# A gated scan with two feed-forward layers: block 1 of layer 1 in seven products, and the making of layer 2's output weights moved one phase on

## The chip, the cores and the metric

The kernel runs on one core of one Trainium2 chip. The metric is device microseconds of one execution, median of several runs; lower is better. A kernel has five engines here: TensorE (PE, matmuls), VectorE (DVE), ScalarE (ACT), GpSimd (POOL), and SyncE (SP), which only issues DMAs. Each engine runs its own instruction stream in order, and semaphores tie the streams together.

## The reference

```python
def _attn_ref(x, f_logit, lower_bound):            # x, f_logit: [2, 6080, 256]
    sig = 1.0 / (1.0 + np.exp(-f_logit))
    f = lower_bound + (1.0 - lower_bound) * sig
    i = 1.0 - f
    for t in range(S):
        h = f[:, t] * h + i[:, t] * x[:, t]
        y[:, t] = h
    return y
def _moe_ref(x, w_in, w_out):                      # w_in [256, 2048], w_out [2048, 256]
    h = np.maximum(x @ w_in, 0.0)
    return h * h @ w_out
def _moe2_ref(x, w_in, w_out):
    h = x @ w_in
    g = np.where(h > 0.0, h, np.exp(np.minimum(h, 0.0)) - 1.0)
    return g @ w_out
# reference = _moe2_ref(_moe_ref(_attn_ref(...).reshape(12160, 256)))
```

## The kernel before, in words

**Tiles.** Time is cut into blocks of 512 steps (11 full blocks and a tail of 448), for both batches at once. Block i of layer 1 is `first(i)`, block n of layer 2 `second(n)`. Each is a phase; phases run in the order first(0), first(1), second(0), first(2), second(1) and so on. Their number is `ph.order`: phase zero is first(0), phase one first(1), phase two second(0), phase three first(2). A phase has 8 pairs (`PAIRS`), each of 256 of the 2048 hidden columns; a pair is a step of the phase.

**Precision.** Each fp32 operand is split into a high part (a rounding copy on ACT) and a low part (a subtraction on DVE or POOL). A product of a 128x128 weight tile with 128x512 data is three matmuls (`triple`, L600 to L605).

**Two ways to multiply up.** The first matmul of a layer takes 2x2 tiles of weights to 2x2 tiles of data. A plain phase (`plain()`, before: phases zero and one) does it in 8 triples a step, 24 matmuls. All others use seven products in the manner of Strassen and Winograd: m1 to m7, 21 matmuls (L688 to L731), with four sums of weights (s1 to s4), which are kept in DRAM and loaded for each pair (`load_sums`, `load_s`), and four sums of the data (t1 to t4). The products land in four PSUM banks (`ring`) and are combined: ACT copies m1 (L1096) and m2 (L1104) out, DVE adds m6, m7, m5, m3 and m4 (L1439 to L1464), and POOL adds m1 to m2's copy (c11, L1747). The second matmul of the layer (`down`) has 8 triples, 24 matmuls, for the pair two steps back, into `acc`. In a phase of seven products, PE alternates product and down: m1, down, m2, down, m6, down, m7, down, m5, down, m3, down, m4, down, down.

**After the products.** Of the pair one step back, ACT does the activation of the half n1 (`n1_of`), then of n0 (`relu_of_n0`, `act_of_n0`), then the high parts (`hi_of_n1` L1075, `hi_of_n0` L1085); DVE the low parts (`lo_of`, L1414). In an ACT step the order is: place a, copy of m1, n1_of, place b, relu_of_n0, copy of m2, act_of_n0, hi_of_n1, place c, hi_of_n0, place d. The places take hosted work for other phases: gates, splits of the next inputs, and the preparation of the weights.

**Preparation of the weights**, once, in phases zero and one. For each pair, SP loads the four quarters of w_in, ACT and DVE split them (`quarters_hi` L922, `quarters_lo` L1316), POOL makes four sums (`sums`, L1591 to L1596), ACT takes their high parts (`sums_hi_of`, L929, place b), POOL their low parts (`sums_lo_of`, L1601), and SP stores all to DRAM. Layer 1's run in phase zero, layer 2's in phase one. The output weights are split on ACT (`weights_hi_out`, L941 and L944) and DVE (`weights_lo_out`); layer 1's stay in SBUF, and layer 2's go to DRAM and are loaded for each pair.

**What holds POOL.** Its add of m1 and m2 (c11, L1747) stands behind `pool.wait_ge(lo_n1, cur.g)`: it waits for DVE's low part of n1 of the pair one step back. ACT's relu_of_n0 of the next step waits for c11, and PE's m3 for the copy of m2 (`pe.wait_ge(m2_kept, cur.s + 1)`).

Of the kernel before, what the change touches and what calls it, by code (L numbers as in the profile page):

```python
# [11 lines left out]
P = 128  # L12
# [3 lines left out]
PAIRS = 8  # L16
# [18 lines left out]
def gated_scan_two_ffn(nc, x, f_logit, lower_bound, w_in1, w_out1, w_in2, w_out2, out):  # L35
# [20 lines left out]
    class Phase:  # L56
# [9 lines left out]
        def plain(self):  # L66
            return isinstance(self.order, int) and self.order < 2

    PLAIN = 2 * PAIRS
# [45 lines left out]
    with ExitStack() as ctx:  # L115
# [122 lines left out]
        q_loaded = [sem(f"q_loaded{v}") for v in range(2)]  # L238
# [90 lines left out]
        def wr_count(layer, p):  # L329
            return W_LOADS[1] * (p // 2 + 1) if layer == 1 else W_LOADS[1] * PAIRS // 2 + W_LOADS[2] * (p + 1)  # L330
# [27 lines left out]
        def _(sp):  # L358
# [45 lines left out]
            def load_raw_out(layer, p):  # L404
# [9 lines left out]
                sp.wait_ge(w_lo, PAIRS - 1 if p == 0 else v)  # L414
                sp.dma_start(o, wout2_v[:, 2 * p:2 * p + 2, :]).then_inc(wr_loaded[0], DMA_INC)
# [68 lines left out]


            QUARTER_AT = {1: 1, 4: 2, 5: 3}

            def phase(ph, after):
# [8 lines left out]
                for p in range(PAIRS):  # L497
                    g = ph.base + p
                    nxt = ahead(p + 2)
                    if known(ph.order, 0):  # L500
                        if p == PAIRS - 1:
                            load_q(ahead(p + 1))
                        if p >= 1:
# [10 lines left out]
                            if p + 3 < PAIRS:  # L514
                                load_raw_in(1, p + 3)
                            elif p + 3 < PAIRS + 2:
                                load_raw_in(2, p + 3 - PAIRS)
                        continue
                    if known(ph.order, 1):
                        if p < PAIRS - 1:  # L520
                            load_q(ahead(p + 1))
                        else:
                            load_s(ahead(p + 1))
                            load_sums(ahead(p + 1))
                        if 1 <= p < PAIRS - 1:
# [9 lines left out]
                        if p in QUARTER_AT:  # L535
                            load_f(2, QUARTER_AT[p])
                            load_x(2, QUARTER_AT[p])
                        continue
                    if known(ph.order, 2) and p == 0:
                        load_s(ahead(1))  # L540
                        load_sums(ahead(1))
                    if known(ph.order, 2) and p == 0:
                        keep_sums(2, PAIRS - 1)
# [1262 lines left out]
```

## Time and profile before

| | |
|---|---|
| Median of 3 runs | 1975.05 us (1974.92 to 1975.56) |
| The profiled execution's own time | 1975.2 us |
| Its span, first to last instruction | 1973.4 us |
| PE busy | 1963.1 us (99%), 8734 matmuls |
| DVE, ACT busy | 1574.9 us (80%), 1511.6 us (77%) |
| POOL busy | 608.8 us (31%) |
| PE's granted clock | 0.999 of full speed over the span |
| PE's part in the chain that ended last | 98% |

Busy PE time overlaps (a matmul's 0.39 us reaches into the next), so the pace of PE is read from the starts of its rows. In the rows of the timeline the first number is the start in us from the span's start, the second the time to the end of the row's last instruction. Phase one begins at about 91.5 us, phase two at 178.5, phase three at 260.1 (from the first row of a phase's matmuls and the pace).

### The profile page before, as it was taken

Reading aid. Unit: us, or ns where it says so; the run is one execution under the profiler, and the core shown is the slowest. Engines: PE = TensorE matmul, PEld = TensorE weight load, DVE = VectorE, ACT = ScalarE, POOL = GpSimd, SP = SyncE. Lnnn points to the kernel's source line nnn. Section 1 sums busy time; section 2 is a strip of 40 time slices with the busy share of each in tenths; the row PEclk is TensorE's granted clock in tenths of the full one; section 3 lists DMA queues with packets and bytes.
Section 4 is the critical chain, followed back from the end, with each engine's and each line's share of the span. In section 5 each row is a group of like instructions: output and inputs, shape, how many; then the busy total and the mean of one; then the engine's idle time right before and its main releaser. Section 6 shows DMA issues by size and latency. Waiting matters only on the chain.

```text
span 1973.4 us, 27926 instructions
## 1 busy us (share of the span) xinstructions
PE 1963.1 (99%) x8734; PEld 1636.4 (83%) x8734; DVE 1574.9 (80%) x1775; ACT 1511.6 (77%) x1826; POOL 608.8 (31%) x506
## 2 busy tenths in 40 slices
PE   8999999999999999999999999999999999999998
PEld 6888888888888888888888888888888888888888
DVE  6656888888888888788888888878888877866887
ACT  7888778778777777777777777778777777767766
POOL 3454323323233232332322323223232232322410
PEclk9999999999999999999999999999999999999999
DMA  6668444444444444354444444434444443443453
GB/s 181 198 213 275 147 147 115 148 137 128 136 146 136 128 137 137 114 157 146 125 129 138 133 137 146 139 107 147 143 125 147 141 126 113 142 133 118 140 172 111
DMA packets 229635, 283.09 MB, mean 143 GB/s; under 512 B 153729, under 2 KB 166018, under 8 KB 229506
## 3 DMA queue, kind: packets, MB, share of 16 engines
q1 hardware_dynamic: 226832, 280.49, 46.4%
q10 hardware_dynamic: 2674, 1.25, 0.2%
q8 instruction: 36, 0.59, 0.1%
q14 instruction: 93, 0.76, 0.1%
HBM read 249.30 MB, written 32.37 MB: 143 GB/s over the span
## 4 chain that ended last, share of the span: by engine, by line
PE 98%; ACT 0%; DMA 0%; DVE 0%; POOL 0%; issue 0%; ACTq 0%; DVEq 0%
PE acc L604 52%; PE ring L604 46%; DMA xb<-in_x_dram 0%; PE acc L756 0%; POOL ee L1601 0%; POOL o_sb L1596 0%; DVE wout L1323 0%; DVE y_raw L1496 0%; ACT xb L1017 0%; ACT hid_hi L1075 0%; ACT xb L1012 0%; ACT xa L1017 0%; DVE t_lo L1502 0%; ACT t_hi L1150 0%; DVE y_raw L1488 0%
## 5 line engine op out<-in xcount | busy, mean ns | idle before, releaser
L604 PE MATMUL acc<-hid_hi,wout 128*128 128x512 f32 (+1 forms) x3072 | 1142.4, 387 | 1.2 <-DVE wout L1323 0.7
L604 PE MATMUL ring<-t_hi,s_w 128*128 128x512 f32 (+1 forms) x2720 | 1035.2, 387 | 1.4 <-DVE t_lo L1502 1.4
L604 PEld LDWEIGHTS acc<-hid_hi,wout 128*128 128x128 f32 x3072 | 576.7, 188 | 115.4 <-issue 1.1
L604 PEld LDWEIGHTS ring<-t_hi,s_w 128*128 128x128 f32 x2720 | 510.6, 188 | 103.4 <-DVE t_lo L1502 1.6
L604 PE MATMUL acc<-hid_lo,wout 128*128 128x512 f32 (+1 forms) x1536 | 594.7, 387 | 0.0
L604 PE MATMUL ring<-t_lo,s_w 128*128 128x512 f32 (+1 forms) x1360 | 526.6, 387 | 0.0
L1747 POOL TENSOR_TENSOR xb<-xb,m_sb 128x512 f32<-128x512 f32 (+1 forms) x176 | 225.7, 1282 | 965.1 <-DVE hid_lo L1414 962.8
L1096 ACT ACTIVATE m_sb<-ring 128x512 f32<-128x512 f32 (+1 forms) x176 | 104.4, 593 | 363.6 <-PE ring L604 345.0
L604 PEld LDWEIGHTS acc<-hid_lo,wout 128*128 128x128 f32 x1536 | 288.4, 188 | 56.5
L604 PEld LDWEIGHTS ring<-t_lo,s_w 128*128 128x128 f32 x1360 | 255.3, 188 | 50.4
L1414 DVE TENSOR_TENSOR hid_lo<-xa,hid_hi 128x1024 fp32r<-128x1024 f32 (+1 forms) x191 | 230.7, 1208 | 82.5 <-ACT hid_hi L1075 82.4
L1414 DVE TENSOR_TENSOR hid_lo<-xb,hid_hi 128x1024 fp32r<-128x1024 f32 (+1 forms) x191 | 241.5, 1264 | 30.4 <-ACT hid_hi L1085 30.4
L1085 ACT ACTIVATE hid_hi<-xb 128x1024 fp32r<-128x1024 f32 (+1 forms) x191 | 200.1, 1048 | 37.5 <-DVE xb L1408 37.0
L1456 DVE TENSOR_TENSOR xa<-ring,u_sb 128x1024 f32<-128x1024 f32 (+1 forms) x176 | 211.9, 1204 | 0.0
L1408 DVE SCALAR_TENSOR_TENSOR xa<-ee,xa 128x1024 f32<-128x1024 f32 (+1 forms) x95 | 115.4, 1215 | 104.9 <-ACT ee L1042 104.9
L1075 ACT ACTIVATE hid_hi<-xa 128x1024 fp32r<-128x1024 f32 (+1 forms) x191 | 198.7, 1040 | 0.5
L1439 DVE TENSOR_TENSOR u_sb<-ring,m_sb 128x512 f32<-128x512 f32 (+1 forms) x176 | 118.4, 673 | 44.1 <-PE ring L604 43.1
L1445 DVE TENSOR_TENSOR u_sb<-ring,u_sb 128x512 f32<-128x512 f32 (+1 forms) x176 | 120.6, 685 | 40.6 <-PE ring L604 28.8
L1408 DVE SCALAR_TENSOR_TENSOR xb<-ee,xb 128x1024 f32<-128x1024 f32 (+1 forms) x95 | 114.9, 1209 | 26.4 <-ACT ee L1065 26.4
L1460 DVE TENSOR_TENSOR xa<-ring,xa 128x512 f32<-128x512 f32 (+1 forms) x176 | 120.7, 686 | 18.3
L1464 DVE TENSOR_TENSOR xb<-ring,u_sb 128x512 f32<-128x512 f32 (+1 forms) x176 | 118.0, 670 | 0.0
L1042 ACT ACTIVATE ee<-ee 128x1024 f32<-128x1024 f32 (+1 forms) x95 | 100.2, 1054 | 3.0
(122 smaller groups left out, 1706.5 us busy)
## 6 DMA issues: line engine op xcount, KB each, us to landing
s_w<-s_kept SPq DMA_DIRECT2D x184, 512.0 KB, 3.8
s_w<-s_kept SPq DMA_DIRECT2D x176, 384.0 KB, 4.1
wout<-w_kept SPq DMA_DIRECT2D x96, 512.0 KB, 4.4
out_dram<-o_sb SPq DMA_DIRECT2D x88, 128.0 KB, 3.5
f_raw<-in_f_logit_dram SPq DMA_DIRECT2D x168, 64.0 KB, 3.5
x_raw<-in_x_dram SPq DMA_DIRECT2D x168, 64.0 KB, 2.7
s_kept<-ee SPq DMA_DIRECT2D x16, 512.0 KB, 5.2
s_kept<-s_w SPq DMA_DIRECT2D x8, 512.0 KB, 3.9
```

The source lines that it names most:

```text
L604: mm = nc.tensor.matmul(out_ap, lhs[a], rhs[b], start=start and t == 0, stop=stop and t == 2)
L1075: nc.scalar.activation(hid_hi[:, pr.par(), 0:2, 0:N], xa[:, pr.par(), :, 0:N], ACT.Copy).then_inc(hi_n1, 1)
L1085: nc.scalar.activation(hid_hi[:, pr.par(), 2:4, 0:N], xb[:, pr.par(), :, 0:N], ACT.Copy).then_inc(hi_n0, 1)
L1096: nc.scalar.activation(m1_sb[:, 0:N], bank("m1", cur), ACT.Copy).then_inc(m1_kept, 1)
L1408: nc.vector.scalar_tensor_tensor(out=x2, in0=ee[:, v, :, 0:pr.N], scalar=1.0, in1=x2, op0=ALU.subtract, op1=ALU.max).then_inc(done, 1)
L1414: nc.vector.tensor_tensor(hid_lo[:, pr.par(), k:k + 2, 0:N], x2, hid_hi[:, pr.par(), k:k + 2, 0:N].bitcast(F32), ALU.subtract).then_inc(do ...
L1439: nc.vector.tensor_tensor(u[:, 0], bank("m6", cur), m1_sb[:, 0:N], ALU.add).then_inc(u2_done, 1)
L1445: nc.vector.tensor_tensor(u[:, 1], bank("m7", cur), u[:, 0], ALU.add).then_inc(u3_done, 1)
L1456: nc.vector.tensor_tensor(t, bank("m5", cur).unsqueeze(1).broadcast_to([P, 2, N]), u, ALU.add).then_inc(u4_done, 1)
L1460: nc.vector.tensor_tensor(t[:, 0], bank("m3", cur), t[:, 0], ALU.add).then_inc(c12_done, 1)
L1464: nc.vector.tensor_tensor(x_n0(cur)[:, 1], bank("m4", cur), u[:, 1], ALU.add).then_inc(c21_done, 1)
L1747: nc.gpsimd.tensor_tensor(t, t, m1_sb[:, 0:N], ALU.add).then_inc(c11_done, 1)
```

## The change

- Phase one, first(1), is no longer plain: its up matmuls are seven products with the loaded sums of layer 1. Its data sums t1 to t4 are made in phase zero, on POOL, their high parts there on ACT (5c, 6b, 6c), and their low parts on DVE (`lo_b1` to `lo_tb1`) instead of POOL. Phase zero's second scan of a quarter moves from place c to b.
- Phase one loads sums and quarters (`load_s`, `load_sums`) as other phases do; `load_q` is gone.
- Layer 2's sums stay in phase one, but on POOL they now stand behind c11: in step p, c11, one hosted operation for the next phase, the low parts of sums p, then the sums of pair p + 1. The hosted operations for second(0) move one pair later (`crowded`).
- Layer 2's output weights are split in phase two: ACT at place a, POOL (no longer DVE) ahead of c11, stored by SP. Down matmuls of phase two use them in their place, without a load. Layer 2's quarters take that tile (`wout2`) in phase one.

The pieces below are, in order: which phases are plain and where layer 2's quarters lie; TensorE; SyncE in phase zero; ScalarE; GpSimd.

```diff
         def plain(self):
-            return isinstance(self.order, int) and self.order < 2
+            return isinstance(self.order, int) and self.order < 1
...
         def q2_new(p):
-            t = (t_lo if p % 2 else t_hi)[1]
-            return t[:, 4:6, :].rearrange("p v s -> p (v s)").rearrange("p (x h m) -> p x h m", h=2, m=P)
+            return wout2[:, p % 2].rearrange("p j h d -> p (j h d)").rearrange("p (x h m) -> p x h m", h=2, m=P)
...
             plain_phase(first(0))
-            plain_phase(first(1))
...
+            phase(first(1))
             phase(second(0))
...
-                        if p == PAIRS - 1:
-                            load_q(ahead(p + 1))
...
+                        if p >= PAIRS - 2:
+                            load_s(nxt)
+                            load_sums(nxt)
...
+                    crowded = known(ph.order, 1)
...
                 if known(ph.order, 1):
                     if place == "a":
                         quarters_hi(2, p)
                     if place == "b":
                         sums_hi_of(2, p)
-                    if place == "d" and p < PAIRS - 1:
-                        weights_hi_out(2, p)
+                if known(ph.order, 2) and place == "a" and p >= 1:
+                    weights_hi_out(2, p - 1)
...
                 if ph.plain():
...
+                    sums(1, p)
+                    if p == 6:
+                        sum_t1(first(1))
+                        sum_t3(first(1))
+                        sum_t2(first(1))
+                        sum_t4(first(1))
+                    sums_lo_of(1, p)
+                    if p == PAIRS - 1:
+                        sums(2, 0)
                     return
-                if nxt is not None and 2 <= p < 7:
+                nxt = inputs_of(ph)
+                crowded = known(ph.order, 1)
+                if nxt is not None and 2 <= p < (8 if crowded else 7):
...
+                if known(ph.order, 2) and p >= 1:
+                    weights_lo_out(p - 1)
...
                 pool.wait_ge(lo_n1, cur.g)
...
                 nc.gpsimd.tensor_tensor(t, t, m1_sb[:, 0:N], ALU.add).then_inc(c11_done, 1)
                 if nxt is not None:
-                    if p == 1:
+                    if p == (2 if crowded else 1):
                         lo_b(nxt)
...
+                if crowded:
+
+                    sums_lo_of(2, p)
+                    if p < PAIRS - 1:
+                        sums(2, p + 1)
```

How the streams move. First POOL in phase one, at pair 2 (before; `o_sb` holds the raw quarters and sums, `ee` the stored form, `z_raw` the data of phase two):

```order
L1594 TENSOR_TENSOR o_sb<-o_sb 128x128 [waits sums_done]
L1596 TENSOR_TENSOR o_sb<-o_sb 128x128 [waits sums_done]
L1615 TENSOR_TENSOR t_lo<-z_raw,t_hi 128x512 [waits t_hb]
L1658 TENSOR_TENSOR z_raw<-z_raw 128x512 [waits t_lb]
L1601 TENSOR_TENSOR ee<-o_sb,ee 128x4x128 [waits sums_hi]
L1591 TENSOR_TENSOR o_sb<-o_sb 128x128 [waits r_loaded1]
```

The same place in the changed kernel, from c11 of pair 2 to c11 of pair 3:

```order
L1723 TENSOR_TENSOR xb<-xb,m_sb 128x512 [waits m1_kept,m2_kept,lo_n1,m6_done]
L1608 TENSOR_TENSOR t_lo<-z_raw,t_hi 128x512 [waits t_hb]
L1594 TENSOR_TENSOR ee<-o_sb,ee 128x4x128 [waits sums_hi]
L1584 TENSOR_TENSOR o_sb<-o_sb 128x128 [waits r_loaded1]
L1585 TENSOR_TENSOR o_sb<-o_sb 128x128
L1587 TENSOR_TENSOR o_sb<-o_sb 128x128 [waits sums_done]
L1589 TENSOR_TENSOR o_sb<-o_sb 128x128 [waits sums_done]
L1642 TENSOR_TENSOR z_raw<-z_raw 128x512 [waits t_lb,m6_done]
L1723 TENSOR_TENSOR xb<-xb,m_sb 128x512 [waits m2_kept,m1_kept,lo_n1]
```

The sums of a pair (L1584 to L1589) now come after the c11 of the pair before, with its wait on lo_n1, one hosted operation and the low parts.

ACT in phase one, at pair 3, before:

```order
L922 ACTIVATE t_lo1<-o_sb 128x3x128 [waits s2_stored1,r_loaded1]
L1012 ACTIVATE xa<-ring 128x1024 [waits lo_n1,up_n1]
L1017 ACTIVATE xa<-xa 128x1024 [waits relu_n1]
L1075 ACTIVATE hid_hi<-xa 128x1024 [waits down_n1,acted_n1]
L929 ACTIVATE ee<-o_sb 128x4x128 [waits sums_stored1,sums_done]
L1012 ACTIVATE xb<-ring 128x1024 [waits lo_n0,up_n0]
```

and in the changed kernel:

```order
L896 ACTIVATE wout2<-o_sb 128x3x128 [waits s2_stored1,r_loaded1]
L1074 ACTIVATE m1_sb<-ring 128x512 [waits c11_done,u2_done,m1_done]
L1008 ACTIVATE xa<-xa 128x1024 [waits c12_done,u4_done]
L1010 ACTIVATE xa<-xa 128x1024 [waits relu_n1]
L903 ACTIVATE ee<-o_sb 128x4x128 [waits sums_stored1,sums_done]
L1029 ACTIVATE xb<-xb 128x1024 [waits c21_done,c11_done]
L1082 ACTIVATE xb<-ring 128x512 [waits lo_n0,m2_done]
```

The copy of the sums (L903, waits for sums_done from POOL) stands ahead of the copy of m2 (L1082), for which PE's m3 waits.

## Rows read from the trace of the kernel before

**Rows 1.** Waits of PE, whole span (waited for: us in total, times, longest).

```profile
PE ring L604 <- DVE t_lo L1502: 1.4, 1, 1.4
...
PE acc L604 <- DVE hid_lo L1414: 0.5, 1, 0.5
```

**Rows 2.** Busy time by window (stretch, its length, each engine): phases one, three.

```profile
91.50:178.50 87.00, 87.00 (x385) 72.05 (x384) 50.77 (x56) 71.75 (x95) 53.71 (x52) 1.00 0.73 239
...
260.10:341.70 81.60, 81.60 (x361) 67.57 (x361) 68.07 (x79) 65.02 (x80) 24.42 (x19) 1.00 0.45 129
```

**Rows 3.** PE timeline, phase three: m1 and m3 of a step, the next m1.

```profile
280.56 0.39 PE L604 MATMUL ring<-t_hi,s_w 128*128 128x512 f32 x1
...
287.36 0.39 PE L604 MATMUL ring<-t_hi,s_w 128*128 128x512 f32 x1
...
290.76 0.39 PE L604 MATMUL ring<-t_hi,s_w 128*128 128x512 f32 x1
```

**Rows 4.** Timeline of ACT in phase three, two steps.

```profile
285.88 0.57 ACT L1104 ACTIVATE xb<-ring 128x512 f32<-128x512 f32 x1
...
287.30 1.04 ACT L1075 ACTIVATE hid_hi<-xa 128x1024 fp32r<-128x1024 f32 x1
...
305.33 1.04 ACT L1051 ACTIVATE xb<-xb 128x1024 f32<-128x1024 f32 x1
306.28 0.58 ACT L1104 ACTIVATE xb<-ring 128x512 f32<-128x512 f32 x1
```

**Rows 5.** Timeline of DVE in phase three.

```profile
288.38 1.22 DVE L1414 TENSOR_TENSOR hid_lo<-xa,hid_hi 128x1024 fp32r<-128x1024 f32 x1 [1.57 <-ACT hid_hi L1075]
...
294.41 1.83 DVE L1291 TENSOR_TENSOR_SCAN y_raw<-gate,carry,x_t 128x256 f32<-128x256 f32 x1
```

**Rows 6.** Timeline of POOL in phase three.

```profile
289.68 1.30 POOL L1747 TENSOR_TENSOR xb<-xb,m_sb 128x512 f32<-128x512 f32 x1 [4.18 <-DVE hid_lo L1414]
290.93 1.30 POOL L1629 TENSOR_TENSOR t_lo<-z_raw,t_hi 128x512 fp32r<-128x512 f32 x1
294.40 1.30 POOL L1629 TENSOR_TENSOR t_lo<-z_raw,t_hi 128x512 fp32r<-128x512 f32 x1 [2.17 <-PE ring L604]
```

**Rows 7.** Timeline of POOL in phases zero and one: low parts and sums.

```profile
61.82 1.29 POOL L1601 TENSOR_TENSOR ee<-o_sb,ee 128x512 fp32r<-128x512 f32 x1 [7.41 <-ACT ee L929]
...
64.83 0.46 POOL L1596 TENSOR_TENSOR o_sb<-o_sb 128x128 f32<-128x128 f32 x1
...
140.97 2.26 POOL L1601 TENSOR_TENSOR ee<-o_sb,ee 128x512 fp32r<-128x512 f32 x1
...
145.25 0.80 POOL L1596 TENSOR_TENSOR o_sb<-o_sb 128x128 f32<-128x128 f32 x1
...
158.09 1.81 POOL L1601 TENSOR_TENSOR ee<-o_sb,ee 128x512 fp32r<-128x512 f32 x1 [0.66 <-ACT ee L929]
...
161.24 1.44 POOL L1596 TENSOR_TENSOR o_sb<-o_sb 128x128 f32<-128x128 f32 x1
```

**Rows 8.** Timeline of DVE in phase one.

```profile
161.14 1.23 DVE L1414 TENSOR_TENSOR hid_lo<-xb,hid_hi 128x1024 fp32r<-128x1024 f32 x1 [2.39 <-ACT hid_hi L1085]
...
165.73 0.54 DVE L1316 TENSOR_TENSOR t_hi<-o_sb,t_hi 128x384 fp32r<-128x384 f32 x1
...
174.38 0.74 DVE L1291 TENSOR_TENSOR_SCAN y_raw<-gate,carry,x_t 128x256 f32<-128x256 f32 x1
```

**Rows 9.** Timeline of ACT, pair 0 of phase one: copy of sums, then relu.

```profile
102.99 0.61 ACT L929 ACTIVATE ee<-o_sb 128x512 fp32r<-128x512 f32 x1
103.51 1.01 ACT L1012 ACTIVATE xb<-ring 128x1024 f32<-128x1024 f32 x1
```

**Rows 10.** Timeline of ACT where phase one ends and two begins.

```profile
181.81 1.06 ACT L1085 ACTIVATE hid_hi<-xb 128x1024 fp32r<-128x1024 f32 x1
182.77 0.58 ACT L1096 ACTIVATE m_sb<-ring 128x512 f32<-128x512 f32 x1
```

**Rows 11.** Timeline of POOL in phase two, a c11 with its idle time.

```profile
217.67 1.30 POOL L1747 TENSOR_TENSOR xb<-xb,m_sb 128x512 f32<-128x512 f32 x1 [2.30 <-DVE hid_lo L1414]
```

More of the change, by code:

```diff
@@ L460, in load_s @@
                 v = pr.par()
-                if known(pr.phase.order, 2):
-                    sp.wait_ge(s2_stored[v], DMA_INC * (pr.p // 2 + 1))
+                if isinstance(pr.phase.order, int) and pr.phase.order < 3:
+                    sp.wait_ge((s1_stored if pr.layer == 1 else s2_stored)[v], DMA_INC * (pr.p // 2 + 1))
                 if isinstance(pr.s, int) and pr.s < 2:
@@ L534, in phase @@
                             keep_sums(2, p - 1)
[L535 to L543, printed above, removed]
+                    if known(ph.order, 2):
+                        if 1 <= p < PAIRS - 1:
+                            load_raw_out(2, p + 1)
+                        if p == 0:
+                            keep_sums(2, PAIRS - 1)
+                        else:
+                            keep_w2(p - 1)
+                    if known(ph.order, 3) and p == 0:
+                        keep_w2(PAIRS - 1)
+                        for v in range(2):
+                            sp.wait_ge(w2_stored[v], DMA_INC * PAIRS // 2)
                     if ph.layer == 1 and not known(ph.i, TAIL):
@@ L842, in set_free @@
             def set_free(ph):
-                if isinstance(ph.order, int) and ph.order < 4:
-                    act.wait_ge(up_n0, ph.base - PAIRS)
-                else:
+                if known(ph.order, 2):
+                    act.wait_ge(up_n0, PLAIN)
+                elif not known(ph.order, 1):
                     act.wait_ge(m4_done, ph.base - PAIRS - PLAIN)
@@ L854, in raw_of @@
                 return z_raw if ph.layer == 2 else y_raw
-            def split_plain_b(ph):
-                raw_ready(ph, False)
-                nc.scalar.activation(t_hi[ph.order % 2][:, 0:4:3, :], raw_of(ph)[:, 0], ACT.Copy).then_inc(t_hb, 1)
             def split_b(ph):
@@ L972, in hosted @@
                 if nxt is not None:
-                    late = ph.plain() or (ph.layer == 2 and known(ph.i, TAIL - 1))
+                    crowded = known(ph.order, 1)
+                    late = crowded or (ph.layer == 2 and known(ph.i, TAIL - 1))
                     if at == ((2, "c") if late else (1, "b")):
@@ L989, in hosted @@
                         tanh(ph.i + 1, 2)
-                    if at == (7, "d") and not ph.plain():
+                    if at == (7, "d"):
                         tanh(ph.i + 1, 3)
-                if known(ph.order, 2):
-                    if at == (0, "c"):
-                        tanh(2, 3)
-                    if at == (0, "d"):
-                        weights_hi_out(2, PAIRS - 1)
                 if known(ph.order, 1):
```

249 lines of the change are left out of this document (108 added, 141 removed).

## The prediction

> **What bounds the kernel now.** I read the waits of PE first, then the busy time by window, then the timelines of single steps. PE waits for others six times in the whole span, all in the first 28 us: the longest is 1.4 us, the shortest shown 0.5 [rows 1]. From there to the end PE is never late: in both windows it is busy for the full stretch, 87.00 of 87.00 and 81.60 of 81.60 us [rows 2]. So every matmul taken away counts, and so does every wait that appears. A step of seven products is 45 matmuls and takes 290.76 - 280.56 = 10.20 us, 0.2267 us a matmul [rows 3]. PE's granted clock is 1.00 in both windows [rows 2], the 2.4 GHz level.
>
> **The gain.** Phase one goes from 48 to 45 matmuls in each of 8 steps: 24 x 0.2267 = **5.4 us less** on PE, and 4390 matmuls stand in the written stream (loop body once) where 4414 did. This counts in full only if the others keep a step of 10.20 us in phase one. Nothing else on PE changes.
>
> **Who has to keep up, and how late they may be.** PE issues m3 287.36 - 280.56 = 6.80 us into a step [rows 3], and m3 waits for ACT's copy of m2. That copy starts at 285.88, 5.32 us in, and takes 0.57 [rows 4], so it may start at 6.23 and has 0.9 us to spare. What matters in phase one is thus the return time R, from the start of one copy of m2 to the next. If R is over 10.20, PE waits the difference at each m3.
>
> **R in the changed phase one.** POOL's sums of pair p + 1 now come after c11 of pair p, and ACT takes them ahead of the copy of m2. So a loop closes through three engines. Its terms:
> - From the copy of m2 to c11. ACT goes on to the high part of n1 (287.30), DVE makes the low part (288.38, 1.22 us), and c11, which waits for it, starts at 289.68 [rows 4 to 6]: 289.68 - 285.88 = 3.80.
> - c11 itself: 290.93 - 289.68 = 1.25 to the next start [rows 6].
> - One hosted operation for phase two, in five of the seven turns (pairs 2 to 6): 1.27, near the 1.30 of rows 6.
> - Low parts of sums p and sums p + 1, five instructions. Three instances: 61.82 to 65.29 = 3.47; 158.09 to 162.68 = 4.59; 140.97 to 146.05 = 5.08 [rows 7].
> - ACT's copy of the sums to its next instruction 0.52 [rows 9], 0.08 for the semaphores, relu_of_n0 to the copy of m2 306.28 - 305.33 = 0.95 [rows 4].
>
> Which of the three instances holds is decided by what DVE does at that time. In rows 5 and 6 a scan and a POOL low part start together at 294.4: POOL's takes its usual 1.30, the scan 1.83 where one takes 0.74 alone [rows 8]. In the instance of 4.59, the last sum takes 1.44 where one takes 0.46 in the first instance, exactly beside DVE's low part at 161.14 [rows 7, 8]. So the two exclude each other, whole instructions at a time. In the changed loop DVE makes the low part of n0 right in this window (1.23), and in pairs 2, 4 and 6 the scans (0.74 each) fall in it too; the quarters (0.54) come near its end [rows 8]. I take 4.6 for pairs 3 and 5, the instance with such overlap, and 4.6 + 0.7 = 5.3 for 2, 4 and 6, near the worst instance. The Trainium skill (SBUF — State Buffer, Who interferes with whom) has a rule for this: a DVE instruction with two SBUF inputs and a GpSimd instruction that reads SBUF exclude each other, and whoever starts first holds the port. By that rule the sum is the one taken here; if they only shared a bandwidth, or not at all, it would be the first rival's below. The trace agrees with the rule at 294.4.
>
> R = 3.80 + 1.25 + 1.27 + 4.6 + 0.08 + 0.52 + 0.95 = 12.5 us for pairs 3 and 5, and 13.2 for 2, 4 and 6. Five turns: 2 x 12.5 + 3 x 13.2 = 64.6 us, where PE's five steps need 51.0. **Excess 13.6 us.**
>
> **Slack before it starts.** Pairs 0 to 2 have no hosted operation behind c11 ahead of them. The copy of m2 in pair 2 starts at 5.32 less the one hosted copy in that step (0.95) plus the copy of the sums 0.52, plus 0.7 because ACT's second copy of `acc` must wait for the end of PE's step 1 and the quarters' copy follows: about 5.6, slack 6.23 - 5.6 = 0.6 us. **Less 0.6.**
>
> **Start of phase one.** Where phase one ends today, ACT's copy of m1 comes 0.96 after hi_of_n0 starts, at 182.77 [rows 10], and ends at 183.35; PE wants it for m5 at 178.5 + 24 x 0.2267 = 183.9. In the changed kernel, two copies stand between them at the start of phase one, some 0.5 + 0.4. That makes it 0.4 late. **Plus 0.4.**
>
> **Edits at nothing.** The work for t1 to t4 in phase zero: POOL had 7.41 us idle ahead of its row at 61.82 [rows 7], and the four sums (4 x 1.3) take the place of three low parts of about the same time; ACT gets two copies of 0.95 and gives one back, over a phase with plain matmuls to wait for. If that cover is gone, the first m5 and m6 of phase one are late. Weights in phase two: ACT's two copies fall where it waits for the next m1. POOL's two subtractions of 256 elements, between 0.45 and 1.30 each by size [rows 6, 7], about 1.5 in all, have 2.30 us idle ahead of c11 [rows 11]. Bounds are 0 and 0.4 a step (both delayed by a DVE instruction of 1.2), and a late c11 has room: it ends at 290.98, 0.2 into the next step, and ACT's relu_of_n0 wants it at 285.88 - 0.95, 4.4 into one [rows 3, 4, 6]. So 0. SP: eight `load_q` go, eight loads each of sums and quarters come; they land in about 4 us and are asked for a step ahead. SP's wait on w_lo stands ahead of the next loads in phase two, which m3 and m4 hold until later anyway. SP's f and x loads are the same in number.
>
> **Sum**: -5.4 + 13.6 - 0.6 + 0.4 = **+8.0 us**. The profiled execution of 1975.2 would be 1983.2; it stands 0.15 above the median of 1975.05, which goes to **1983.0**. About 0.2% (4 us) is what a measurement of this kernel can tell from no change.
>
> **Bounds.** Low: 3.47 in all five turns, R = 11.3: excess 56.7 - 51.0 = 5.7, less slack 0.9: -5.4 + 4.8 = -0.6, and if the 3.47, which has a slowed operation in it, were 0.3 shorter, -2.1: 1973. High: the worst instance 5.08 in pairs 3 and 5 and a scan on top in the others (5.8): R = 12.95 and 13.7, excess 16.0, and 1.4 for the starts of phases one and two: +12: 1987. I lean to neither end, since DVE's low part must fall in this window.
>
> **Rivals.**
> 1. *The loop closes, but DVE and POOL do not meet in it*: R is 11.3 in all turns. Then about -0.6 to -2.1 us: 1973.5, no measurable change. For it: instances of 3.47 are the commonest in phase zero. Against: there DVE has no products to combine and meets POOL with one instruction; in phase one the low part of n0 follows c11 by a fixed order, and the POOL chain behind c11 is some 6 us long.
> 2. *The loop does not decide*: the sums are ready before ACT asks for them, because the wait for lo_n1 is met earlier than in phase three, or m3's copy has more slack than I read. It needs R under 10.2, so that 3.80 and the hosted operation shrink by 1.2 us together even with sums of 3.47. Then the ACT and DVE loop decides, which holds 10.20 in phase three and would get the 0.52 on top: -5.4 + 0.5: 1970.1, faster. ACT's own work speaks half against it: its busy time is 65.0 of 81.6 in phase three and 71.8 of 87.0 in phase one [rows 2].
> 3. *More waits than the loop*: the stored sums of pair 7 are late for the first activation of phase two, or PE's granted clock falls to 1.2 GHz in the gaps. The gaps would be 2 to 3 us at each m3. With either, some 6 us more: 1989, slower. No row shows such gaps in the main part, so this stays small.
>
> That the change does nothing is excluded: the matmuls are gone from the stream.
>
> **Chances.** Forecast 0.57, rival 1 0.22, rival 2 0.13, rival 3 0.08. The forecast case itself spans 1978 to 1987. Faster by over 0.2% is rival 2: 0.13. Within 0.2%, 1971.1 to 1979.0: rival 1 and the low edge of the forecast, 0.25. Slower: 0.62. Range: 1973 to 1987; it leaves out rival 2 and most of rival 3.
>
> **What would show it.** In the profile after: PE busy in phase one clearly short of its window, with a wait of PE on ACT's copy of m2 in pairs 3 to 7, some 2 to 3 us each. ACT's copy of the sums idle before it, released by POOL's last sum. c11 starts about 3.8 after the copy of m2. Phase one takes about 95 us where 81.6 would do. Phases two and on as before. If PE shows no wait there, the loop was misread and rival 2 holds; if PE's waits are there but of 1 us, rival 1; if they are on loads or on `t_lo`, my edits at nothing were wrong.

## The result, and the profile after

The changed kernel takes **1984.72 us** (median of 6 runs, 1983.23 to 1985.60); the kernel before took 1974.99 beside it (6 runs). The ratio is 1.0048, interval 1.0037 to 1.0058: slower by 9.7 us. The profiled execution took 1985.6 us with a span of 1983.9; that of before took 1975.2. The six executions of the changed kernel lie in two groups, three from 1983.23 to 1983.88 and three from 1985.55 to 1985.60, and the profiled one is of the upper group. What follows on the profile is about that execution.

The waits of PE, whole span, which answer to [rows 1] (waited for: us in total, times, longest):

```profile
PE ring L592 <- ACT xb L1082: 9.4, 5, 2.2
PE ring L592 <- DMA s_w<-s_kept: 2.0, 1, 2.0
PE ring L592 <- DVE t_lo L1495: 1.4, 1, 1.4
```

Two lines are new: five waits for ACT's copy of m2 (`xb`, L1082), together 9.4 us, and one for a load of `s_w`, 2.0 us. All six fall in phase one or at its start. From the page: PE's busy time in 8710 matmuls, and the chain of waits, in which POOL, ACT and a DMA now have a share:

```profile
PE 1962.0 (99%) x8710; PEld 1632.1 (82%) x8710; DVE 1608.1 (81%) x1803; ACT 1519.4 (77%) x1844; POOL 642.7 (32%) x531
...
PE 94%; POOL 2%; ACT 2%; DVE 1%; DMA 1%; issue 1%; SPq 0%; ACTq 0%; POOLq 0%; DVEq 0%
```

The busy time by window (stretch, its length, each engine with its instructions, granted clock of PE, DMA share, GB/s): phase one, then two and three.

```profile
91.76:188.21 96.45, 85.08 (x361) 68.43 (x361) 68.91 (x80) 72.84 (x97) 57.85 (x61) 0.98 0.65 212
188.21:270.67 82.46, 82.44 (x361) 67.23 (x360) 71.94 (x75) 66.81 (x86) 44.67 (x36) 1.00 0.49 168
270.67:352.27 81.60, 81.60 (x361) 67.57 (x360) 69.06 (x79) 65.66 (x82) 27.00 (x22) 1.00 0.45 130
```

The first stretch runs from 91.76, where PE is done with phase zero and could start its next matmul, to the first matmul of phase two; the others from the first matmul of their phase to that of the next. Each holds the 360 matmuls of a phase of seven products (the counts also take in one that reaches in from before). Phase one of the changed kernel is 96.45 us long with 85.08 of PE, where phase one had 87.00 of 87.00 [rows 2]. Phase two takes 82.46, 0.86 over the 81.60 that it took before, in small delays that leave PE busy nearly all the time. Phase three takes 81.60, and from its start to the end both kernels take 1713.2 us.

The loop is seen in one turn, from the copy of m2 in pair 2 to that in pair 3. ACT first (start, duration, instruction, idle time before it and what ended that; they answer to [rows 4, 9]):

```profile
121.59 0.57 ACT L1082 ACTIVATE xb<-ring 128x512 f32<-128x512 f32 x1
...
132.85 0.63 ACT L903 ACTIVATE ee<-o_sb 128x512 fp32r<-128x512 f32 x1 [3.08 <-POOL o_sb L1589]
...
134.33 0.58 ACT L1082 ACTIVATE xb<-ring 128x512 f32<-128x512 f32 x1
...
145.01 0.63 ACT L903 ACTIVATE ee<-o_sb 128x512 fp32r<-128x512 f32 x1 [2.66 <-POOL o_sb L1589]
```

And POOL in the same turn (this view and the next answer to [rows 5 to 8]):

```profile
125.45 1.29 POOL L1723 TENSOR_TENSOR xb<-xb,m_sb 128x512 f32<-128x512 f32 x1 [5.56 <-DVE hid_lo L1407]
126.71 1.29 POOL L1608 TENSOR_TENSOR t_lo<-z_raw,t_hi 128x512 fp32r<-128x512 f32 x1
127.96 1.68 POOL L1594 TENSOR_TENSOR ee<-o_sb,ee 128x512 fp32r<-128x512 f32 x1
129.61 1.44 POOL L1584 TENSOR_TENSOR o_sb<-o_sb 128x128 f32<-128x128 f32 x1
131.01 0.85 POOL L1585 TENSOR_TENSOR o_sb<-o_sb 128x128 f32<-128x128 f32 x1
...
132.35 0.47 POOL L1589 TENSOR_TENSOR o_sb<-o_sb 128x128 f32<-128x128 f32 x1
```

DVE at that time:

```profile
124.09 1.23 DVE L1407 TENSOR_TENSOR hid_lo<-xa,hid_hi 128x1024 fp32r<-128x1024 f32 x1 [1.32 <-ACT hid_hi L1053]
...
127.17 1.39 DVE L1266 TENSOR_TENSOR_SCAN y_raw<-gate,carry,x_t 128x256 f32<-128x256 f32 x1
...
129.06 1.67 DVE L1407 TENSOR_TENSOR hid_lo<-xb,hid_hi 128x1024 fp32r<-128x1024 f32 x1
130.66 0.94 DVE L1266 TENSOR_TENSOR_SCAN y_raw<-gate,carry,x_t 128x256 f32<-128x256 f32 x1
```

POOL's c11 starts 3.86 after the copy of m2: it waited for DVE's low part of n1 (124.09), and that for ACT's high part. The hosted low part starts 1.26 later, and the low part of the sums with the four sums takes 127.96 to 132.82, 4.86 us. ACT has been idle 3.08 us when the last sum releases it at 132.85, and its copy of m2 comes 1.48 later, 12.74 after the last one. What stretches the chain is DVE: POOL's 1.68 at 127.96 (1.30 alone) lies beside the scan at 127.17, its 1.44 at 129.61 (0.46 alone) beside the low part of n0 at 129.06, its 0.85 at 131.01 beside the scan at 130.66. DVE pays too: 1.39 and 0.94 for scans of 0.74, 1.67 for a low part of 1.22. The ends of the rows show one after the other rather than both at half pace: DVE's low part, which starts first, ends at 130.73, and POOL's sum of 0.46, begun beside it at 129.61, ends at 131.05, 0.32 after it. The turn of pair 3 is the same with 4.31 for the chain of sums: 12.16.

The start of phase one, on PE, and the loads on SP's queue:

```profile
91.53 0.39 PE L592 MATMUL ring<-t_hi,s_w 128*128 128x512 f32 x1
93.92 0.60 PE L592 MATMUL ring<-t_hi,s_w 128*128 128x512 f32 x1 [2.00 <-DMA s_w<-s_kept]
94.32 0.63 PE L592 MATMUL ring<-t_lo,s_w 128*128 128x512 f32 x1
```

```profile
87.91 0.43 SPq L464 DMA_DIRECT2D s_w<-s_kept  x1
```

PE waits 2.0 us for `load_s` of pair 0 (L464), asked for at 87.91 and landed 5.96 later, at 93.87. Then the matmuls come 0.43 us apart instead of 0.227. The granted clock says why (same columns as the windows above): 0.50, which is the 1.2 GHz level, and 1.00 again from 97.7.

```profile
94.30:97.30 3.00, 3.00 (x8) 2.31 (x7) 0.00 (x0) 2.94 (x4) 2.48 (x4) 0.50 1.02 415
97.70:100.70 3.00, 3.00 (x15) 2.47 (x14) 2.52 (x4) 2.56 (x6) 0.46 (x2) 1.00 0.33 136
```

Where the 10.4 us of the profiled executions went (1985.6 - 1975.2): 24 matmuls fewer, -5.4; the five waits for the copy of m2 +10.7, read as the spacing of PE's starts over 0.2267 (it holds the restart of PE as well as the 9.4 of waiting); the wait for the load +2.2 in the same measure; the 3.4 us at 1.2 GHz +1.7; small delays of PE in phase two +0.8. Sum +10.0. Another 0.24 is there before phase one: the last matmul of phase zero starts at 91.53, and at 91.29 in the kernel before.

### The profile page after: what moved, and what is told of

It reads as the page before. It is cut to its first block, busy times and chain, and to the rows that moved or that the text cites. A ratio compares the mean times of both kernels' runs of the same rounds, so it can differ in the third digit from the quotient of the medians.

```text
span 1983.9 us, 27952 instructions
## 1 busy us (share of the span) xinstructions
PE 1962.0 (99%) x8710; PEld 1632.1 (82%) x8710; DVE 1608.1 (81%) x1803; ACT 1519.4 (77%) x1844; POOL 642.7 (32%) x531
## 4 chain that ended last, share of the span: by engine, by line
PE 94%; POOL 2%; ACT 2%; DVE 1%; DMA 1%; issue 1%; SPq 0%; ACTq 0%; POOLq 0%; DVEq 0%
PE acc L592 50%; PE ring L592 44%; POOL ee L1594 1%; ACT hid_hi L1053 0%; POOL xb L1723 0%; ACT xb L1029 0%; DVE hid_lo L1407 0%; SPq L368 0%; DMA s_w<-s_kept 0%; POOL o_sb L1584 0%; DMA xb<-in_x_dram 0%; ACT xb L1040 0%; POOL o_sb L1589 0%; POOL o_sb L1585 0%; POOL o_sb L1587 0%
## 5 line engine op out<-in xcount | busy, mean ns | idle before, releaser
L1723 POOL TENSOR_TENSOR xb<-xb,m_sb 128x512 f32<-128x512 f32 (+1 forms) x184 | 236.2, 1284 | 978.7 <-DVE hid_lo L1407 976.1
L1074 ACT ACTIVATE m_sb<-ring 128x512 f32<-128x512 f32 (+1 forms) x184 | 109.2, 594 | 355.7 <-PE ring L592 339.3
L592 PEld LDWEIGHTS acc<-hid_lo,wout 128*128 128x128 f32 x1536 | 288.5, 188 | 56.7
L1407 DVE TENSOR_TENSOR hid_lo<-xb,hid_hi 128x1024 fp32r<-128x1024 f32 (+1 forms) x191 | 242.0, 1267 | 11.3 <-ACT hid_hi L1063 11.2
L1449 DVE TENSOR_TENSOR xa<-ring,u_sb 128x1024 f32<-128x1024 f32 (+1 forms) x184 | 221.6, 1204 | 0.0
L1401 DVE SCALAR_TENSOR_TENSOR xa<-ee,xa 128x1024 f32<-128x1024 f32 (+1 forms) x95 | 115.5, 1216 | 106.8 <-ACT ee L1020 106.8
L1432 DVE TENSOR_TENSOR u_sb<-ring,m_sb 128x512 f32<-128x512 f32 (+1 forms) x184 | 123.8, 673 | 50.8 <-PE ring L592 49.5
L1438 DVE TENSOR_TENSOR u_sb<-ring,u_sb 128x512 f32<-128x512 f32 (+1 forms) x184 | 126.1, 685 | 44.4 <-PE ring L592 31.8
L1453 DVE TENSOR_TENSOR xa<-ring,xa 128x512 f32<-128x512 f32 (+1 forms) x184 | 126.2, 686 | 19.1
L1401 DVE SCALAR_TENSOR_TENSOR xb<-ee,xb 128x1024 f32<-128x1024 f32 (+1 forms) x95 | 116.7, 1228 | 23.7 <-ACT ee L1043 23.7
L1457 DVE TENSOR_TENSOR xb<-ring,u_sb 128x512 f32<-128x512 f32 (+1 forms) x184 | 123.3, 670 | 0.0
L1082 ACT ACTIVATE xb<-ring 128x512 f32<-128x512 f32 (+1 forms) x184 | 105.5, 573 | 0.0
```

Source lines behind the costliest of these rows:

```text
L592: mm = nc.tensor.matmul(out_ap, lhs[a], rhs[b], start=start and t == 0, stop=stop and t == 2)
L1074: nc.scalar.activation(m1_sb[:, 0:N], bank("m1", cur), ACT.Copy).then_inc(m1_kept, 1)
L1401: nc.vector.scalar_tensor_tensor(out=x2, in0=ee[:, v, :, 0:pr.N], scalar=1.0, in1=x2, op0=ALU.subtract, op1=ALU.max).then_inc(done, 1)
L1407: nc.vector.tensor_tensor(hid_lo[:, pr.par(), k:k + 2, 0:N], x2, hid_hi[:, pr.par(), k:k + 2, 0:N].bitcast(F32), ALU.subtract).then_inc(do ...
L1432: nc.vector.tensor_tensor(u[:, 0], bank("m6", cur), m1_sb[:, 0:N], ALU.add).then_inc(u2_done, 1)
L1438: nc.vector.tensor_tensor(u[:, 1], bank("m7", cur), u[:, 0], ALU.add).then_inc(u3_done, 1)
```

## The experiments

Two theories. **The loop**: ACT copies layer 2's sums ahead of its copy of m2, so POOL's sums stand in a loop: POOL's sums, ACT's copy of them and then its copy of m2 and the high part of n1, DVE's low part of n1, POOL's c11 and the next sums. Its length R sets five steps. PE is not in the loop; it waits for it once a turn, at m3. **The rival**: ACT and DVE, which got more work in phase one, are just too full, or the start of phase one (load and clock) carries much of the loss, and the place of one copy matters little. The kernel before took 1974.99 beside the changed one, 1975.16 beside e1 to e4 and 1975.23 beside e5 to e8. One view repeats: the starts of ACT's copy of m2. Five turns are from that in pair 2 to that in pair 7.

| kernel | us (runs) | ratio to before, interval | five turns | waits for the copy of m2 |
|---|---|---|---|---|
| changed | 1984.72 (6) | 1.0048 [1.0037, 1.0058] | 184.03 - 121.59 = 62.44 | 9.4, five |
| e1_copy_at_c | 1974.05 (11) | 0.9994 [0.9985, 1.0003] | 170.93 - 119.48 = 51.45 | none |
| e2_sums_first | 1974.69 (11) | 0.9998 [0.9989, 1.0007] | 171.42 - 119.57 = 51.85 | 0.3, one |
| e3_hosted_last | 1981.18 (7) | 1.0030 [1.0019, 1.0041] | 178.84 - 121.22 = 57.62 | 3.6, three |
| e4_loads_early | 1985.11 (5) | 1.0050 [1.0037, 1.0064] | 181.91 - 119.54 = 62.37 | 9.3, five |
| e5_less_lo | 1978.35 (11) | 1.0015 [1.0006, 1.0025] | 176.71 - 119.64 = 57.07 | 4.1, five |
| e8_double_lo | 1991.27 (5) | 1.0082 [1.0069, 1.0096] | 187.88 - 119.52 = 68.36 | 12.2, five |
| e6_copies_later | 1972.45 (11) | 0.9986 [0.9977, 0.9995] | 169.88 - 118.45 = 51.43 | none |
| e7_weights_first | 1971.71 (11) | 0.9982 [0.9973, 0.9991] | 169.08 - 117.62 = 51.46 | none |

### Opening the loop on ACT: e1_copy_at_c

```
-                    if place == "b":
+                    if place == "c":
                         sums_hi_of(2, p)
```

Place b is ahead of relu_of_n0 and the copy of m2; place c is behind hi_of_n1, ahead of hi_of_n0. No work is added or taken.

> In phase one ACT copies the sums at place c, behind the copy of m2 and hi_of_n1, instead of place b; ACT has the same work. Theory 1 (the loop from the copy of m2 over lo_n1, c11, the hosted operation and the sums on POOL back to ACT's copy of the sums): the five waits of PE on the copy of m2, 10.7 us with their restarts, go away, since nothing ahead of the copy of m2 waits for POOL's sums any more: about 1974 us, and no row of PE waiting on xb L1082. Theory 2 (ACT has too much work in phase one for steps of 10.20 us): the order changes nothing in the amount, waits of 1 to 2 us stay in pairs 3 to 7: 1983 to 1985.

Measured: 1974.05, 10.7 us under the changed kernel. The waits of PE have no line of the copy of m2:

```profile
PE ring L592 <- ACT xb L990: 0.6, 1, 0.6
PE ring L592 <- ACT m_sb L1074: 0.5, 1, 0.5
```

On ACT the copy of the sums now comes behind the copy of m2 and has no idle time ahead of it; POOL's sums are as slow as before and nobody waits:

```profile
119.48 0.58 ACT L1082 ACTIVATE xb<-ring 128x512 f32<-128x512 f32 x1
...
122.37 0.62 ACT L903 ACTIVATE ee<-o_sb 128x512 fp32r<-128x512 f32 x1
...
125.85 1.68 POOL L1594 TENSOR_TENSOR ee<-o_sb,ee 128x512 fp32r<-128x512 f32 x1
```

ACT and DVE have as much to do as in the changed kernel (1519.2 and 1609.7 us busy over the span, where it has 1519.4 and 1608.1), so the rival "too full" falls: between a gain of 5.4 and a loss of 9.7 lie 15.1 us, and the order alone carried 10.7 of them. The five turns are 11.0 shorter. Phases one and two of e1 take 84.36 and 83.25 us, so 4.4 over 163.2 is left in them; it is what e6 and e7 go after. The wait for `s_w` is 0.2 here and no stretch is at 1.2 GHz, but the shorter wait is no effect of the edit: the loads stand where they did, and PE waits for them 2.0, 1.3, 2.0, 0.2 and 1.4 in the changed kernel, e2, e3, e5 and e8. That wait differs from one execution to the next. The two profiled executions with a wait of 2.0, those of the changed kernel and of e3, are also the slowest of their kernels. So the start of phase one is dearer in these two profiles than in the medians, by an amount that no run here gives.

### Opening it on POOL: e2_sums_first

```
+                if crowded:
+                    sums_lo_of(2, p)
+                    if p < PAIRS - 1:
+                        sums(2, p + 1)
                 pool.wait_ge(lo_n1, cur.g)
...
-                if crowded:
-
-                    sums_lo_of(2, p)
-                    if p < PAIRS - 1:
-                        sums(2, p + 1)
```

> In phase one POOL does the low parts and the next sums ahead of c11 and its wait on lo_n1, so the same loop is cut at the other end. The sums (3.1 to 4.7 us of POOL) would run from ACT's copy of the sums to about the time when lo_n1 is met. Theory 1: the waits on the copy of m2 go: 1974 to 1976, the worse end if c11 comes late by DVE's port. Theory 2 (too much work on ACT): 1983 to 1985 as in the changed kernel.

Measured: 1974.69. One wait of 0.3 for the copy of m2 is left, and 1.3 for `s_w`, so that wait is there without the loop. Two different cuts of the same loop, one on ACT and one on POOL, end within 0.7 us of each other. That is the loop theory's forecast, and a theory about either engine alone would not give it.

### Shortening it by one instruction: e3_hosted_last

The hosted operation of POOL (1.27) goes behind the sums; the rest is as in the changed kernel.

```
                 nc.gpsimd.tensor_tensor(t, t, m1_sb[:, 0:N], ALU.add).then_inc(c11_done, 1)
+                if crowded:
+                    sums_lo_of(2, p)
+                    if p < PAIRS - 1:
+                        sums(2, p + 1)
                 if nxt is not None:
...
```

> In phase one the hosted operation behind c11 moves behind the sums, so the loop gets shorter by one POOL instruction of 1.25 us but stays closed. Theory 1: the return time R falls from 12.2 and 12.7 to about 10.9 and 11.4, each of the five waits of PE shrinks by 1.2, some 6 us in all: 1978.5. If the loop's length were not what sets the waits (theory 2), they stay: 1984.7.

Measured: 1981.18, 2.7 us above the expectation. Four of five turns did as expected: 11.38, 10.69, 10.68 and 11.31 us. The turn of pair 4 took 13.56. ACT waits 3.23 us there for POOL's t3 of phase two's data (L1649), itself a hosted operation, now behind the sums. ACT's split of it stands ahead of its copy of m2 in pair 5, so the work that I moved out of the loop came back in by another wait, 2.2 us over a turn of its kind (both engines, in order of time):

```profile
152.35 0.73 POOL L1589 TENSOR_TENSOR o_sb<-o_sb 128x128 f32<-128x128 f32 x1
...
153.05 1.29 POOL L1649 TENSOR_TENSOR z_raw<-z_raw 128x512 f32<-128x512 f32 x1
...
154.43 1.06 ACT L859 ACTIVATE t_hi<-z_raw 128x1024 fp32r<-128x1024 f32 x1 [3.23 <-POOL z_raw L1649]
...
155.39 0.61 ACT L903 ACTIVATE ee<-o_sb 128x512 fp32r<-128x512 f32 x1
```

PE's longest wait is 3.1 us there, and a second stretch at 1.2 GHz follows it. The move did the same once more in pair 7. The last low part of phase two's data (L1632) now stands behind POOL's low part of the last sums, and PE's m6 of phase two's first step waits for it (`inputs_in(t_ltb, 1, 2)`). The view names no one for that wait, but PE goes on 0.10 us after the row of POOL ends:

```profile
185.16 2.25 POOL L1632 TENSOR_TENSOR t_lo<-z_raw,t_hi 128x512 fp32r<-128x512 f32 x1
...
187.51 0.47 PE L592 MATMUL ring<-t_hi,s_w 128*128 128x512 f32 x1 [1.55 <-issue]
```

With its restart that is 1.8 us. The two together are 4.0, and the profiled execution (1982.28, the slowest of the seven) is 3.8 above the expectation. The miss is mine: I costed the move by its length and did not look who reads what it makes.

### The start of phase one: e4_loads_early

```
                             if p == 6:
+                                load_s(nxt)
+                                load_sums(nxt)
                                 load_f(2, 0)
                                 load_x(2, 0)
...
-                        if p >= PAIRS - 2:
+                        if p == PAIRS - 1:
                             load_s(nxt)
                             load_sums(nxt)
```

> SP issues pair 0's loads of sums and quarters for phase one ahead of the f and x loads of pair 6 in phase zero. Theory 3 (the 2.0 us wait at the start of phase one is these loads standing behind eight others in SP's queue): it goes, and with it the 1.7 us that the eight matmuls at the 1.2 GHz level behind it cost. But ACT's copy of m1 ended at 99.25 where PE would then ask for it at 97.2, so about 2 us come back as a wait at m5: 1982.5 to 1983. If nothing stood behind it: 1981. If the loads are slow wherever they are issued: 1984.7.

Measured: 1985.11, no gain where 2 us were expected. The waits of PE (lines shifted by 2) show what stepped in:

```profile
PE ring L594 <- ACT xb L1084: 9.3, 5, 2.2
...
PE ring L594 <- ACT xb L992: 1.2, 1, 1.2
...
PE ring L594 <- ACT m_sb L1076: 0.5, 1, 0.5
```

The loads are asked for 7 us earlier and nobody waits for them, but PE then waits 1.2 us for ACT's `xb` (L992) and 0.5 for its copy of m1. ACT makes that `xb` behind its copy of layer 1's last sums, at 93.71 with 1.61 of idle time ahead of it, released by POOL's last sum. So POOL is late there. Both waits are there in e1 and e5 as well (0.6 and 0.5 us), where PE waited only 0.2 for the load. And the stretch at 1.2 GHz did not go: it moved behind the last of the five waits (0.55 over this window):

```profile
183.10:186.40 3.30, 3.30 (x10) 2.56 (x9) 2.15 (x3) 3.27 (x6) 0.68 (x1) 0.55 0.99 349
```

So the load hid a second wait close behind it, and in these two profiles the stretch at 1.2 GHz is paid in one place or the other. ACT's last copy of m2 in the loop does come 2.1 us earlier (181.91 for 184.03); the stretch takes 1.7 of that back.

### Less beside POOL: e5_less_lo

DVE's low part of n0 in phase one is made for 16 columns only. The rest of the low parts for that half of phase one's hidden values is left out of the computation.

```
-                    lo_of(last, 2, x_n0(last), hi_n0, lo_n0)
+                    if known(ph.order, 1):
+                        dve.wait_ge(hi_n0, last.g + 1)
+                        nc.vector.tensor_tensor(hid_lo[:, last.par(), 2:4, 0:16], x_n0(last)[:, :, 0:16],
+                                                hid_hi[:, last.par(), 2:4, 0:16].bitcast(F32),
+                                                ALU.subtract).then_inc(lo_n0, 1)
+                    else:
+                        lo_of(last, 2, x_n0(last), hi_n0, lo_n0)
```

> In phase one DVE makes only 16 of the 512 columns of the low part of n0 (the rest of hid_lo keeps old numbers, so the low parts of half of phase one's hidden values are left out); everything else as in the changed kernel. Theory 1a (POOL's chain behind c11 is stretched because it and DVE's two-input instructions exclude each other): that instruction takes about 1.1 us out of the loop, low parts and sums take 3.2 to 3.8 us in place of 4.3 to 4.9, R falls by about 1.1 in each of five turns, the waits by 5 us: 1979.5. Theory 1b (the chain takes this long by itself, DVE has no part in it): unchanged, 1984.7.

Measured: 1978.35. No instruction of the loop was touched; DVE only has no 1.2 us instruction beside POOL's sums any more. The same chain on POOL:

```profile
126.01 1.69 POOL L1600 TENSOR_TENSOR ee<-o_sb,ee 128x512 fp32r<-128x512 f32 x1
127.66 0.46 POOL L1590 TENSOR_TENSOR o_sb<-o_sb 128x128 f32<-128x128 f32 x1
128.07 0.85 POOL L1591 TENSOR_TENSOR o_sb<-o_sb 128x128 f32<-128x128 f32 x1
...
129.43 0.46 POOL L1595 TENSOR_TENSOR o_sb<-o_sb 128x128 f32<-128x128 f32 x1
...
137.73 1.29 POOL L1600 TENSOR_TENSOR ee<-o_sb,ee 128x512 fp32r<-128x512 f32 x1
138.99 0.45 POOL L1590 TENSOR_TENSOR o_sb<-o_sb 128x128 f32<-128x128 f32 x1
...
140.36 0.47 POOL L1595 TENSOR_TENSOR o_sb<-o_sb 128x128 f32<-128x128 f32 x1
```

It takes 126.01 to 129.89 = 3.88 us instead of 4.86, the rest being the scans, and in the next turn 137.73 to 140.83 = 3.10 instead of 4.31, where no row is slowed. The turns are 11.77, 10.93, 11.71, 10.94 and 11.72 us: 1.0 to 1.2 shorter each, as the chain is, and 5.4 together; the time is 6.4 lower, part of it the start of phase one. That is the part of the rule on DVE and POOL in the prediction (the Trainium skill, SBUF — State Buffer, Who interferes with whom): with the overlapping DVE instruction gone, a sum that took 1.44 takes 0.46.

### Lengthening it: e8_double_lo

POOL makes the low part of the sums twice in pairs 2 to 6.

```
+                    if 2 <= p < 7:
+                        t = sums_new(p)
+                        pool.wait_ge(sums_hi, PAIRS + p + 1)
+                        nc.gpsimd.tensor_tensor(t[:, :, 1, :].bitcast(F32R), r_slot(2, p)[:, NQ:NQ + NS], t[:, :, 0, :],
+                                                ALU.subtract).then_inc(twice, 1)
+                        pool.wait_ge(twice, p - 1)
                     sums_lo_of(2, p)
```

> The changed kernel with POOL's low parts of the sums made twice in pairs 2 to 6 of phase one. Theory 1: each of the five return times grows by one such instruction, 1.3 to 1.7 us, and the full amount lands on PE: 6.5 to 8.5 us more, 1991 to 1993. If POOL had room in the loop (something else ends last): less than 2 us more.

Measured: 1991.27, 6.55 over the changed kernel. The copies of m2 (ACT, same columns as above):

```profile
119.52 0.58 ACT L1083 ACTIVATE xb<-ring 128x512 f32<-128x512 f32 x1
...
133.50 0.58 ACT L1083 ACTIVATE xb<-ring 128x512 f32<-128x512 f32 x1
```

The turns are 13.98, 13.27, 13.92, 13.27 and 13.92 us, 1.1 to 1.2 longer each, 5.9 together. So is the chain on POOL: from 125.90 to 131.98, 6.08 us where it was 4.86, and 5.45 for 4.31 in the next turn. That is a little less than the 1.3 of such an instruction alone; the rows of the chain lie against other rows of DVE now. What POOL's chain grows by comes out at PE nearly 1:1, though POOL is 32% busy over the span.

### Both ends open: e6_copies_later and e7_weights_first

e6 is e1 with e4's loads, and with layer 1's last copy of sums at place c too:

```
-                    if place == "b":
+                    if place == ("c" if p == PAIRS - 1 else "b"):
                         sums_hi_of(1, p)
```

e7 is e6, and in phase two POOL makes the low parts of the output weights ahead of its hosted operation:

```
                 crowded = known(ph.order, 1)
+                if known(ph.order, 2) and p >= 1:
+                    weights_lo_out(p - 1)
+                if known(ph.order, 3) and p == 0:
+                    weights_lo_out(PAIRS - 1)
                 if nxt is not None and 2 <= p < (8 if crowded else 7):
...
```

> The copy of layer 2's sums at place c, pair 0's loads for phase one early, and the copy of layer 1's last sums (pair 7 of phase zero) at place c as well, behind relu_of_n0. In the kernel with the first edit alone PE still waited 0.6 us on the relu of n0 and 0.5 us on the copy of m1 at the start of phase one, both behind that copy of the sums, which waited 1.6 us for POOL. Theory (POOL is late at the end of phase zero and ACT stands behind it): these go, 1973.0. If something else holds them (the work on ACT there): 1974.

> As e6_copies_later, and in phase two POOL makes the low parts of the output weights ahead of the hosted operation instead of behind it. In the changed kernel phase two took 0.8 us over 81.6: POOL's weights met DVE's elu of n0 (1.81 us in place of 1.23), c11 and the copies behind it came late. Placed first they fall where DVE is idle. If that is the cause, 0.8 us less than e6_copies_later: 1972.2. If the 0.8 comes from ACT's copies of the weights: no difference.

Measured: 1972.45 and 1971.71. The two edits at the start of phase one are worth 1974.05 - 1972.45 = 1.6 us together; which of them brings it, the loads or the copy, no run here separates. The weights' place is worth 0.7. The intervals of the ratios overlap, but the runs do not (e6 from 1972.18, e7 up to 1972.10), and the difference lies in phase two. The windows of e6 (phase two) and e7 (phases one and two) show it:

```profile
175.14:258.39 83.25, 82.98 (x361) 67.03 (x360) 72.98 (x76) 66.85 (x86) 45.02 (x36) 1.00 0.52 175
...
91.68:174.34 82.66, 82.26 (x362) 67.34 (x361) 70.52 (x79) 72.87 (x97) 58.56 (x60) 1.00 0.70 222
174.34:256.91 82.57, 82.31 (x362) 67.26 (x360) 71.25 (x77) 66.35 (x86) 45.68 (x36) 1.00 0.53 178
```

Phase two goes from 83.25 to 82.57, and phase one of e7 takes 82.66 where it took 96.45 in the changed kernel.

e7 is **3.5 us faster than before** and 13.0 faster than the change as it was made, with the same instructions in another order. The matmuls alone are worth 5.4; the missing 1.9 lie in these two phases, which are 2.0 over 163.2 together. Three short delays of PE make 1.2 of it (0.40 behind the matmul at 96.9, 0.33 behind that at 154.6, 0.43 behind that at 175.7 us).

## Why the prediction was right

Forecast 1983.0, measured 1984.72, inside 1973 to 1987 and in the forecast case; slower was the likeliest side. The mechanism, the loop, was right; the closeness of the number owes something to luck. Point by point:

- **PE bounds and the gain is 5.4.** It held: 8710 matmuls, and from phase three on the same time as before; e7 keeps 3.5 of it once the waits are gone. One reading was off: the last of the six waits of the kernel before ends at 37.03, not in the first 28 us. Nothing rests on it.
- **The loop.** It held in mechanism. c11 was forecast 3.80 after the copy of m2 and came 3.81 to 3.86 after it. The chain of low part and sums was forecast 4.6 and 5.3 and took 4.31 and 4.86. R was forecast 12.5 and 13.2 and was 12.2 and 12.7. The waits of PE were forecast at 2 to 3 us each and were 1.63 to 2.19, and phase one was forecast at about 95 us and took 96.45. The five turns took 62.4 where I had 64.6, and the excess over 51.0 was 11.4 for 13.6. The term sized too large is that of the sums, by 0.3 in its base (the instance of 4.59 with its overlap [rows 7], where 4.31 came) and by 0.15 in what the scans add (0.7, where 0.55 came). e1, e2, e5 and e8 show the loop from four sides: open it on ACT, on POOL, shorten it, lengthen it.
- **DVE and POOL exclude each other.** It held: e5 shows that they hold each other up, and the rows at 129.06 and 129.61 above that it is one after the other. Rival 1 (no meeting, R of 11.3) is nearly what e5 makes, with five turns of 57.07 where I had 56.7. It took 1978.35 and not my 1973.5, which left out what the start of phase one and phase two cost.
- **Start of phase one, forecast 0.4.** The 0.4 was for ACT's copy of m1, and that wait was there where the load left room for it: 0.5 in e1, e4 and e5. What failed is a term that I had put at nothing, the loads: 2.2 for the wait and 1.7 for the clock behind it. The prediction's own sign for that, a wait of PE on loads, came. I had written that the sums and quarters land in about 4 us and are asked for a step ahead. They took 6.0 us here, and were issued behind eight loads of f and x at 87.91, only 3.85 us ahead of the matmul at 91.76 that wants them. I also put t1 to t4 at 1.3 each; beside DVE they took 2.21, 1.62, 2.09 and 2.15, so POOL was late with layer 1's last sums, as e4's wait for `xb` shows. The rows of POOL:

```profile
79.35 2.21 POOL L1642 TENSOR_TENSOR y_raw<-y_raw 128x512 f32<-128x512 f32 x1 [1.68 <-DVE t_lo L1305]
81.64 1.62 POOL L1649 TENSOR_TENSOR y_raw<-y_raw 128x512 f32<-128x512 f32 x1
83.41 2.09 POOL L1657 TENSOR_TENSOR y_raw<-y_raw 128x512 f32<-128x512 f32 x1
85.58 2.15 POOL L1664 TENSOR_TENSOR y_raw<-y_raw 128x512 f32<-128x512 f32 x1
```

- **Weights in phase two, forecast 0 with bounds of 0 to 0.4 a step.** Between the bounds: 0.8 in all, in steps 2, 3, 5 and 6 of phase two (0.1 to 0.3 each). In one of them DVE's part of n0's activation (L1401) takes 1.81, starting at 216.34 beside POOL's weights (215.63), c11 starts at 219.36, and ACT's copy of m1 waits 0.83 for it. e7 took 0.7 back.
- **Rival 3 came in part.** The granted clock did fall to 1.2 GHz in a gap, once, for 1.7 us. The stored sums of pair 7 were not late. I had it as an alternative to the forecast; it came on top of it.

In the sum of 8.0 the start is 3.5 too small and phase two 0.8, and the loop 2.3 too large (13.6 - 0.6 = 13.0, where PE's starts show 10.7): 8.0 + 3.5 + 0.8 - 2.3 = 10.0. Being 1.7 us off is better than the terms were: 4.3 too little and 2.3 too much happened to offset each other.

## What to carry to other kernels

Where in-order engines wait for each other in a ring, and the way around the ring is longer than the work of any one of them, the time per step is the time around the ring, whatever the busy shares are. An engine outside it, as PE here, only waits. So when work is moved into a spare engine, ask in which position of its neighbour's stream its result is taken, and walk the ring from one copy to the same copy a step later, with durations from rows that overlap as the new order will. Then move the taking, not the making: a one-line move of a 0.6 us copy was worth 10.7 us here. And before moving an instruction back, see who reads it, in this phase and the next (e3), and before removing a wait, see what is late just behind it (e4).

## What the hardware showed that was not expected

The granted clock fell to 1.2 GHz inside a stream of which PE was busy 99%, in stretches of 3.4 us with the matmuls 0.43 us apart; in the changed kernel that cost 1.7 us. The kernel before, e1, e2, e5, e6 and e7 had none in phase one; the changed kernel and e4 had one, e3 two, e8 three. Each began behind a wait of PE, but not every wait had one: the changed kernel had its one behind the wait of 2.0 for the load and none behind the waits for the copy of m2, of which the longest was 2.2; e4, without the wait for the load, had its one behind the fifth of those. The four waits of 3 us in e3 and e8 (2.99 to 3.42) each had one behind them. What decides between two waits of about 2.2 no run here settles. Nor does each cost its 1.7: in e8 two of the three fall inside turns of the loop, from 135 and from 162 us. Both turns take 13.27, which is 1.1 more than the same turns of the changed kernel (12.16), while the three turns without such a stretch are 1.2 longer. There PE had to wait for the loop anyway, and a slower PE did not lengthen the loop: one more sign that PE is not in it.

The loads of `s_w` at the start of phase one, issued at the same place in six kernels (all but e4, e6 and e7), made PE wait anything from 0.2 to 2.0 us.
